# Relaying the orders of three engines and the places of woven attention pairs in a fused attention and two-FFN kernel

## The reference, cut to what matters

```python
def _attn_ref(q, k, v):                       # q, k, v: (8, 8, 576, 64)
    ...                                       # nine chunks of 64 rows for each head
    scores = scale * np.matmul(q_c, k_c.transpose(0, 1, 2, 4, 3))
    scores = scores - np.max(scores, axis=-1, keepdims=True)
    attn = np.exp(scores)
    attn = attn / (np.sum(attn, axis=-1, keepdims=True) + 1e-09)
    out = np.matmul(attn, v_c)

def _moe_ref(x, w_gate, w_val, w_out, rms_g): # x: (4608, 512), F = 1536
    rms = np.sqrt(np.mean(x * x, axis=-1, keepdims=True) + 1e-06)
    xn = x / rms * rms_g
    g = xn @ w_gate
    silu = g * (1.0 / (1.0 + np.exp(-g)))
    return (silu * (xn @ w_val)) @ w_out

def _moe2_ref(x, w_in, w_out):                # F = 2048
    h = x @ w_in
    g = h * np.clip(h + 3.0, 0.0, 6.0) / 6.0
    return g @ w_out
```

## Time and profile before

| | us |
|---|---|
| median of 3 runs | 1653.3 |
| lowest, highest | 1642.41, 1655.88 |
| the profiled execution, its own time | 1644.85 |
| its span | 1643.1 |

### The profile page before, as it was taken

One profiled execution on the slowest core, in us unless ns is written; L12 is line 12 of the kernel. 1 busy time (PEld: TensorE's weight loads), 2 busy tenths in 40 slices (PEclk: granted clock), 3 DMA queues, 4 the chain that ended last, 5 costly groups with the idle time before them and its releaser, 6 DMA issues.

```text
span 1643.1 us, 29732 instructions
## 1 busy us (share of the span) xinstructions
PE 1603.6 (98%) x11335; PEld 1568.2 (95%) x11337; DVE 1046.2 (64%) x1441; ACT 858.8 (52%) x1341; POOL 783.7 (48%) x774
## 2 busy tenths in 40 slices
PE   7899999999999999999999999999999999999998
PEld 5688999899999999999999999999999999999998
DVE  4878877868754446755454776665666865455454
ACT  4666766654644444644444565554655654434432
POOL 2543442459876564423240377777676631231231
PEclk9999999999999999999999999999999999999999
DMA  9777777644565655989987856647658986776674
GB/s 181 156 191 170 173 188 168 162 131 155 175 233 198 207 194 197 373 308 315 309 309 279 299 209 239 230 174 251 220 183 287 378 269 202 218 229 212 212 228 118
DMA packets 335646, 366.88 MB, mean 223 GB/s; under 512 B 186256, under 2 KB 299152, under 8 KB 332304
## 3 DMA queue, kind: packets, MB, share of 16 engines
q1 hardware_dynamic: 321584, 334.69, 64.8%
q0 software_dynamic: 8800, 28.85, 5.1%
q10 hardware_dynamic: 5120, 1.44, 0.5%
HBM read 200.80 MB, written 164.10 MB: 222 GB/s over the span
## 4 chain that ended last, share of the span: by engine, by line
PE 86%; SPq 4%; DMA 2%; DVE 2%; issue 2%; POOL 2%; ACT 2%; DVEq 0%; ACTq 0%; POOLq 0%
PE bx L989 14%; PE by L989 14%; PE by L990 14%; PE by L991 14%; PE bx L990 14%; PE bx L991 14%; DMA hl_b<-h_scratch 2%; SPq L583 1%; SPq L576 1%; PE att L958 1%; PE att L967 1%; PE att L914 1%; DVE tx L1523 1%; PE att L937 1%; SPq L590 0%
## 5 line engine op out<-in xcount | busy, mean ns | idle before, releaser
L989 PE MATMUL by<-tx,wr 128*128 128x384 f32 x840 | 285.4, 340 | 4.1 <-ACT vb L1201 2.5
L989 PE MATMUL bx<-tx,wr 128*128 128x384 f32 x840 | 285.5, 340 | 2.6 <-ACT gb L1201 1.2
L991 PE MATMUL bx<-tx,wr 128*128 128x384 f32 x840 | 281.0, 335 | 0.0
L991 PE MATMUL by<-tx,wr 128*128 128x384 f32 x840 | 280.9, 334 | 0.0
L990 PE MATMUL bx<-tx,wr 128*128 128x384 f32 x840 | 280.8, 334 | 0.0
L990 PE MATMUL by<-tx,wr 128*128 128x384 f32 x840 | 280.8, 334 | 0.0
L1574 DVE TENSOR_TENSOR hl_d<-hl_d 128x1536 fp32r<-128x1536 f32 x84 | 147.4, 1788 | 90.1 <-ACT hl_d L1273 90.1
L1892 POOL DMA_DIRECT2D out_dram<-ot x128 | 70.4, 558 | 248.1 <-DVE ot L1597 245.6
L1574 DVE TENSOR_TENSOR hl_b<-hl_b 128x1152 fp32r<-128x1152 f32 x84 | 117.5, 1414 | 106.7 <-ACT hl_b L1273 106.2
L1273 ACT ACTIVATE hl_d<-hl_d 128x1536 fp32r<-128x1536 f32 x84 | 123.3, 1486 | 112.6 <-DMA hl_d<-u_scratch 112.6
L989 PEld LDWEIGHTS by<-tx,wr 128*128 128x128 f32 x840 | 157.7, 188 | 7.6 <-issue 2.8
(11 more groups left out here) (200 smaller groups left out, 3769.6 us busy)
## 6 DMA issues: line engine op xcount, KB each, us to landing
hl_d<-u_scratch SPq DMA_DIRECT2D x84, 768.0 KB, 4.4
hl_b<-h_scratch SPq DMA_DIRECT2D x84, 576.0 KB, 5.8
u_scratch<-ut SPq DMA_DIRECT2D x48, 576.0 KB, 3.7
h_scratch<-ht SPq DMA_DIRECT2D x36, 576.0 KB, 3.5
u_scratch<-ub SPq DMA_DIRECT2D x96, 192.0 KB, 2.7
u_scratch<-ub SPq DMA_DIRECT2D x48, 384.0 KB, 2.5
h_scratch<-vb SPq DMA_DIRECT2D x72, 192.0 KB, 3.2
h_scratch<-vb SPq DMA_DIRECT2D x36, 384.0 KB, 3.1
```

The costliest lines, as they stand in the source:

```text
L989: pe.matmul(dst, w_hi, m_hi, start=start, stop=False, skip_group_check=not opens)
L991: return pe.matmul(dst, w_lo, m_hi, start=False, stop=stop, skip_group_check=not opens)
```

## The change

What TensorE does before the first product is kept. The orders of ScalarE, VectorE and GpSimd around it are relaid; so are the places of pairs 6 to 17, the tables of weight units 2 to 5 and of the operand fills. Unit 3's remainder goes from VectorE to GpSimd. In all woven pairs the shift of the scores stands one slot later and the norm one slot earlier. Loads of q and k for the later pairs start three slots later. In the first lines of SyncE's program q and k of pairs 8 and 9 go ahead of both V loads, and unit 2's raw weights ahead of one V load and of a store.

```diff
--- before.py
+++ after.py
@@ -324,7 +324,7 @@
         return 4 * m + place + 1 if m < B0 else 4 * B0 + 8 * (m - C0) + 2 * place + st + 1
 
 
-    V_C, V_C_SLOT = 11, 28
+    V_C, V_C_SLOT = 11, 27
 
     def qk_buf(n):
         n2 = n // 2
@@ -340,10 +340,10 @@
         return (qk_a, qk_c, qk_b)[which], n % 2 * D, (q_loaded[which], full), (k_loaded[which], full)
 
 
-    QK_FIRST = {5: (5, 2), 6: (10, 2), 7: (27, 2), 8: (41, 2)}
+    QK_FIRST = {5: (3, 2), 6: (9, 2), 7: (27, 4), 8: (44, 4), 9: (56, 4)}
 
     def qk_slots(n2):
-        first, each = QK_FIRST.get(n2, (at_slot_of(2 * n2 - 4, SC) + 4, 1))
+        first, each = QK_FIRST.get(n2, (at_slot_of(2 * n2 - 4, SC) + 7, 1))
         return [first + i // each if i < 14 else first + i - 14 if each == 1 else first + i // each for i in range(16)]
 
     def v_buf(n):
@@ -367,12 +367,12 @@
 
         return 3 * f - 1 if f <= 12 else C0 + 4 * (f - 12) - 1
 
-    SECOND_FILL = {8: 0, 10: 1, 14: 2, 15: 3, 16: 4, 21: 5, 22: 6}
+    SECOND_FILL = {6: 0, 11: 1, 13: 2, 16: 3, 17: 4, 20: 5, 22: 6}
 
     def filled_at(f, slot):
 
 
-        at_slot = SECOND_FILL if f == 1 else {4: 0, 10: 1, 11: 2, 16: 3, 18: 4, 20: 5, 22: 6} if f < 6 else {3: 0, 5: 1, 7: 2, 9: 3, 11: 4, 13: 5, 15: 6}
+        at_slot = SECOND_FILL if f == 1 else {5: 0, 8: 1, 12: 2, 14: 3, 17: 4, 19: 5, 21: 6} if f < 6 else {3: 0, 5: 1, 7: 2, 9: 3, 11: 4, 13: 5, 15: 6}
         return at_slot.get(slot)
 
 
@@ -458,8 +458,8 @@
 
 
     S_FIRST = NG
-    EARLY = {6: (-6, -3, 1, 7), 7: (0, 3, 8, 12), 8: (7, 9, 14, 20), 9: (12, 15, 21, 24), 10: (18, 23, 26, 31), 11: (24, 28, 33, 37), 12: (32, 37, 39, 44), 13: (40, 43, 46, 50), 14: (45, 49, 52, 57), 15: (51, 56, 59, 63), 16: (58, 62, 64, 68), 17: (63, 68, 70, 76)}
-    AFTER = {7: 5, 8: 1, 11: 5, 12: 5, 25: 5, 20: 1, 24: 1, 33: 1, 29: 5, 30: 1, 15: 5, 17: 3, 18: 3, 23: 5, 32: 5, 28: 3, 13: 3, 26: 3, 16: 3, 22: 1, 34: 1, 19: 5, 21: 5, 27: 3}
+    EARLY = {6: (-6, -3, 5, 7), 7: (2, 5, 9, 12), 8: (7, 11, 14, 21), 9: (14, 18, 22, 25), 10: (20, 25, 28, 32), 11: (26, 32, 33, 36), 12: (34, 37, 40, 45), 13: (40, 42, 47, 51), 14: (46, 48, 53, 57), 15: (49, 53, 59, 63), 16: (55, 62, 64, 69), 17: (64, 67, 71, 75)}
+    AFTER = {7: 5, 8: 5, 11: 5, 12: 3, 25: 3, 20: 3, 24: 5, 33: 5, 29: 5, 30: 5, 15: 3, 17: 3, 18: 3, 23: 5, 32: 3, 28: 5, 13: 3, 26: 3, 16: 5, 22: 5, 34: 3, 19: 5, 21: 3, 27: 3, 6: 1, 9: 3, 14: 3, 10: 1, 31: 3}
     SC, TR, AT, XX = 0, 1, 2, 3
 
     def at_slot_of(n, piece):
@@ -505,21 +505,22 @@
         return sum(16 * 8 * len(runs_out(s, a)) for s in range(NSB) for a in range(2) if s % 2 == parity and s // 2 < times)
 
 
-    FIRST_SUMS = {4: XT3, 9: XT4}
-    FIRST_HI = {3: 4, 8: 6}
-    FIRST_LO = {6: 4, 8: 6}
-    SECOND_SUMS = {9: XT1, 10: XT2, 12: XT3, 13: XT4}
+    FIRST_SUMS = {3: XT3, 7: XT4}
+    FIRST_HI = {7: 4, 9: 6}
+    FIRST_LO = {7: 4, 10: 6}
+    SECOND_SUMS = {7: XT1, 11: XT2, 12: XT3, 13: XT4}
 
 
     RAW_AT = {6: (14, 9), 7: (14, 10), 8: (16, 11), 9: (16, 13), 10: (18, 11), 11: (18, 13), 12: (19, 12), 13: (20, 2), 22: (34, 0)}
-    RAW_FIRST_AT = {3: (0, 0), 4: (0, 8), 5: (1, 1)}
-    SUMS_AT = {2: (0, 1), 3: (0, 9), 4: (0, 12), 5: (1, 5), 6: (15, 9), 7: (15, 11), 8: (17, 1), 9: (17, 9), 10: (19, 1), 11: (19, 4)}
-    HI_AT = {2: ((0, 3), (0, 4)), 3: ((0, 9), (0, 10)), 4: ((1, 2), (1, 2)), 5: ((1, 9), (1, 11)),
+    RAW_FIRST_AT = {3: (0, 0), 4: (0, 7), 5: (0, 13)}
+    SUMS_AT = {2: (0, 2), 3: (0, 9), 4: (1, 0), 5: (1, 7), 6: (15, 9), 7: (15, 11), 8: (17, 1), 9: (17, 9), 10: (19, 1), 11: (19, 4)}
+    HI_AT = {2: ((0, 2), (0, 3)), 3: ((0, 8), (0, 11)), 4: ((1, 0), (1, 2)), 5: ((1, 8), (1, 10)),
              6: ((16, 2), (16, 3)), 7: ((16, 4), (16, 6)), 8: ((18, 7), (18, 8)), 9: ((18, 9), (18, 10)),
              10: ((19, 6), (19, 7)), 11: ((19, 8), (19, 9))}
-    LO_AT = {2: ((0, 6), (0, 6)), 3: ((0, 9), (0, 12)), 4: ((1, 4), (1, 4)), 5: ((1, 11), (1, 13)),
+    LO_AT = {2: ((0, 2), (0, 6)), 4: ((1, 4), (1, 4)), 5: ((1, 11), (1, 12)),
              6: ((16, 3), (16, 5)), 7: ((16, 6), (16, 8)), 8: ((18, 8), (18, 9)), 9: ((18, 10), (18, 12)),
              10: ((19, 7), (19, 8)), 11: ((19, 9), (19, 10))}
+    LO_POOL_AT = {3: ((0, 9), (0, 12))}
     STAGE_AT = {}
     U_B = 21
     for u in range(UB, U_B + 1):
@@ -753,11 +754,11 @@
                 load_first_v(n // 2 - 1)
             if n in (5, 7):
                 load_raw_a((n - 5) // 2)
+        load_qk(4)
         load_v(NG)
+        load_raw_a(2)
         load_v(NG + 1)
-        load_qk(4)
         store_x(0, 0)
-        load_raw_a(2)
 
         for m in range(0, 18):
             s, j = m // 3, m % 3
@@ -1333,19 +1334,19 @@
                 weight_hi(0, n - 3)
             if n == 5:
                 fill_hi(0, 0)
+        norm_rows(S_FIRST - 2)
+        weight_hi(1, 0)
+        mean_square(S_FIRST - 1)
         copy_k(S_FIRST + 1)
+        norm_rows(S_FIRST - 1)
         exponentials(S_FIRST)
-        norm_rows(S_FIRST - 2)
-        mean_square(S_FIRST - 1)
-        weight_hi(1, 0)
-        norm_rows(S_FIRST - 1)
+        weight_hi(1, 1)
+        fill_hi(0, 5)
         fill_hi_early(1)
-        fill_hi(0, 5)
+        fill_hi(0, 1)
+        fill_hi(0, 2)
         copy_probsT(S_FIRST)
-        weight_hi(1, 1)
-        fill_hi(0, 1)
         fill_hi_early(2)
-        fill_hi(0, 2)
         fill_hi(0, 3)
 
         for m in range(B0):
@@ -1364,7 +1365,7 @@
                 n = woven(m, slot, AT, 2)
                 if n is not None:
                     mean_square(n)
-                n = woven(m, slot, AT, 4)
+                n = woven(m, slot, AT, 3)
                 if n is not None:
                     norm_rows(n)
                 n = woven(m, slot, SC, 2)
@@ -1532,6 +1533,8 @@
             if u == 1 and part == 0:
 
                 dve.wait_ge(w_lo, part_no(0, 1))
+            if u - 1 in LO_POOL_AT and part == 0:
+                dve.wait_ge(w_lo, part_no(u - 1, 1))
             dve.wait_ge(w_hi, part_no(u, part))
             dve.tensor_tensor(dst[:, :, LO], blocks_of(u, part), dst[:, :, HI].bitcast(F32), ALU.subtract).then_inc(w_lo, 1)
 
@@ -1634,17 +1637,17 @@
             if n > 0:
                 scale_attention(n - 1)
         shift_scores(S_FIRST)
-        copy_q(S_FIRST + 1)
+        fill_lo(0, 0)
         evict_x(S_FIRST - 3)
         scale_attention(S_FIRST - 1)
-        fill_lo(0, 0)
         evict_x(S_FIRST - 2)
+        copy_q(S_FIRST + 1)
         weight_lo(1, 0)
+        evict_x(S_FIRST - 1)
+        weight_lo(1, 1)
+        fill_lo(0, 5)
         fill_lo_early(1)
-        evict_x(S_FIRST - 1)
-        fill_lo(0, 5)
         fill_lo(0, 1)
-        weight_lo(1, 1)
         fill_lo_early(2)
         fill_lo(0, 2)
         fill_lo(0, 3)
@@ -1660,14 +1663,15 @@
                     gated(m - 1, H21)
                 if m > 0 and slot == 1:
                     gated(m - 1, H11)
+                n = woven(m, slot, SC, 1)
+                if n is not None and n + 1 < NN and next_transposed_after(n) == 1:
+                    transpose_qk(n + 1)
+                n = woven(m, slot, SC, 2)
+                if n is not None:
+                    shift_scores(n)
                 n = woven(m, slot, AT, 1)
                 if n is not None:
                     scale_attention(n)
-                n = woven(m, slot, SC, 1)
-                if n is not None and n + 1 < NN and next_transposed_after(n) == 1:
-                    transpose_qk(n + 1)
-                if n is not None:
-                    shift_scores(n)
                 if m > 0 and slot == 3:
                     gated(m - 1, H22)
                 if m > 0 and slot == 4:
@@ -1796,6 +1800,8 @@
 
         def weight_lo(u, part):
             dst = parts_to(u, part)
+            if u > 0 and part == 0:
+                pool.wait_ge(w_lo, part_no(u - 1, 1))
             pool.wait_ge(w_hi, part_no(u, part))
             pool.tensor_tensor(dst[:, :, LO], blocks_of(u, part), dst[:, :, HI].bitcast(F32), ALU.subtract).then_inc(w_lo, 1)
 
@@ -1905,15 +1911,15 @@
         inverse_rms(1)
         sums(0)
         inverse_rms(2)
+        inverse_rms(3)
         weight_lo(0, 0)
         weight_lo(0, 1)
-        inverse_rms(3)
+        inverse_rms(4)
         sums(1)
-        inverse_rms(4)
+        x_sum_early(XT1)
         inverse_rms(5)
-        x_sum_early(XT1)
+        x_sum_early(XT2)
         x_sum(0, XT1)
-        x_sum_early(XT2)
         x_sum(0, XT2)
 
         for m in range(B0):
@@ -1939,6 +1945,8 @@
                     x_sum(f, slot - 8)
                 for u in units_at(SUMS_AT, m, slot):
                     sums(u)
+                for u, part in parts_at(LO_POOL_AT, m, slot):
+                    weight_lo(u, part)
                 if m == B0 - 2 and slot in (1, 4):
                     pool.wait_ge(prod, prod_no(m - 1, 6, 1))
                     load_block(0, slot // 4)
```

## The result

The changed kernel took 1643.5 us in the median of 21 runs (1639.4 to 1650.4), the kernel before 1650.0 in 21 runs beside it (1642.4 to 1655.9). The ratio is 0.9958, with a 95% interval of 0.9947 to 0.9969: a gain of 5 to 9 us. Two profiled executions can't show it: this one of the changed kernel took 1645.49 (span 1643.7), and the one of before 1644.85 (span 1643.1), a quick draw of its kernel. So spans are no guide here; I compare stretches between the same product slots.

What follows compares the result with a forecast made beforehand. TensorE, busy 98% of the span, was taken as the bound, leaving 39.5 us of idle. Step 0 (-2.2), steps 1 to 5 (-0.6) and 6 to 17 (-4.5) sum to -7.3 from a mean of 1649.1: 1642 us, range 1631 to 1655.

Steps and rivals of the forecast that it cites:

- Steps 6 to 17: Later blocks: new fill, norm and shift places remove waits on rows, evictions and accumulators; gain 4.5 us, bounds -5.6 and +2.
- I leave 1.1 for what is late next: Steps 6 to 17: of 5.6 us of idle addressed, 1.1 was kept for the next late thing.
- the transpose at slot 12: Steps 6 to 17: nearest new victim if operand 1's early rounding holds ScalarE up to 1.9 us; over one us spare.
- Step 0: First woven step: stalls removed against new costs, ending 2.2 us early; bounds -5 to +2.
- The two plain stalls: Step 0: TensorE's 2.55 us before slot 7 and 1.00 before pair 8's probabilities, both to go.
- Term (2): Step 0, slot 2: operand 1's remainder behind a split part, start 53.7 instead of 53.13, a loss of 1.9 us.
- Term (3): Step 0, pair 7's probabilities: unit 2's sums from 53.7, remainder 58.8, transpose 60.8; 0.6 us late at slot 6.
- Steps 1 to 5: Pairs' new distances: idle falls from 5.2 to 4.6 us, pair 13 worst at 1.4; gain 0.6, bounds -4 and +4.
- (a): Rival, steps 0 to 17: nearly all addressed idle clears, only four floors remain; -14 us, 1635; chance 0.20.
- (b): Rival: only the later part pays, step 0 gives nothing, steps 1 to 5 lose; -2 us, 1647; chance 0.13.
- (c): Rival: weight chain bounds step 0 if unit 2's sums end after about 59 us; +5 us, 1654; chance 0.10.
- (d): Rival, whole change: moved orders are off the chain except at named stalls; 0 within 1 us, 1649; chance 0.07.

Runs made afterwards that it cites:

- before_again: The kernel before, unchanged, profiled a second time; 1647.3 us in its one run.
- late_only: The kernel before with only the parts of the change that act from step 6 on; 1646.5 us, ratio 0.9985 to the kernel before.
- fill1_10: The changed kernel with operand 1 of blocks 2 to 5 rounded at slot 10 instead of 8; 1639.6 us, ratio 0.9956 to the kernel before.
- unit2_later: The changed kernel with weight unit 2's rounding and remainder moved from slots 2 and 3 to 4 and 5; 1641.2 us, ratio 0.9962 to the kernel before.
- clock run: unit2_later with ten filler matmuls ahead of the attend of slot 1, to keep TensorE busy; 1640.5 us, ratio 0.9966 to the kernel before.
- fill5_later: The changed kernel with operand 5's rounding and remainder behind operand 3's instead of ahead of operand 1's; 1641.4 us, ratio 0.9972 to the kernel before.
- tr13_44: The changed kernel with the transpose of pair 13's probabilities at slot 44 instead of 42; 1641.4 us, ratio 0.9953 to the kernel before.
- best: The changed kernel with fill5_later, fill1_10, tr13_44 and pair 9's rows transposed one slot later; 1640.3 us, ratio 0.9971 to the kernel before.
- after_again: The changed kernel, unchanged, run once more; 1641.4 us, ratio 0.9971 to the kernel before.
- both_later: The changed kernel with the moves of both unit2_later and fill5_later; 1642.3 us, ratio 0.9977 to the kernel before.

## Why the prediction was right, and where it was not

**The number.** 1642 was forecast and 1643.5 measured; the gain over the kernel before beside it was 6.5 us against 7.3. Most of the parts behind it came out smaller: the traces place 3.2 us of it, so that the number came this near is in part luck. Of the signs of being wrong one came, pair 7's transpose later than 62. TensorE's idle in steps 0 to 5 was 10.1 us, under the 12.4, and it waited for no transfer. "The clock is no lever here" was read off one trace; before_again and late_only, with the old order in step 0, have half clock there.

**Steps 6 to 17: -4.5 forecast, -3.2 measured**, in every trace that has them. The mechanism held: the longer waits on rows went and so did the late evictions (one of 0.3 us is left). The step that failed is "I leave 1.1 for what is late next"; it was 2.4. I had looked for it at "the transpose at slot 12"; it came at slot 13 of steps 8 and 11, on a combination behind the remainder. fill1_10 shows it by taking 2.1 us away. The cause I had named, operand 1's early rounding, was right; its victim was VectorE's combination, not ScalarE's exponential.

**Step 0: -2.2 forecast; -0.54 in the first traces of the two kernels and -0.35 in the second.** The forecast holds the 0.5 of a later slot 0, so for the step's own length it is -2.7. The two plain stalls went as said, but the 2.55 us was dear only in some executions: it was 1.29 in before_again and 0.95 in late_only, where the slots ahead of it had run at half clock. Term (2), slot 2 at 53.7, was 54.57. VectorE's timeline of the kernel after, ahead of it:
```profile
51.03 1.50 DVE L1524 TENSOR_TENSOR tx<-xr,tx 128x768 fp32r<-128x768 f32 x1
52.45 1.21 DVE L1529 TENSOR_TENSOR tx<-xt,tx 128x512 fp32r<-128x512 f32 x1
53.57 0.94 DVE L1524 TENSOR_TENSOR tx<-xt,tx 128x256 fp32r<-128x256 f32 x1
...
58.24 2.47 DVE L1539 TENSOR_TENSOR wr<-w_raw_a,wr 128x1024 fp32r<-128x1024 f32 x1 [0.31 <-ACT wr L1187]
```
Term (3) had pair 7's transpose at 60.8. The sums began at 53.07 (53.7 forecast) and the remainder at 58.24, but it took 2.47 us where I had reckoned 1.2, having begun inside a GpSimd sum (57.39 to 59.63); in unit2_later, with GpSimd idle, it took 1.22. The transpose came at 62.75, past the 62 that I had given as wrong. The row of 2.11 us that bears on this stood in the earlier trace rows, and I let it weigh on operand 6 alone. The Trainium skill, SBUF — State Buffer, Who interferes with whom, lets a VectorE operation with both inputs in SBUF and a GpSimd one that reads SBUF exclude each other; the runs agree, with 1.21 against 2.84 us for one remainder. And slots 2 and 3, which I had priced at full clock, took 4.5 us; but the clock run shows that at full clock there the next wait takes most of that back. Slot 8 came at 67.23, not 65.4, and step 1 at 76.39, not 75. So the term of this part that failed is the remainder's length in (3), 1.2 for 2.47.

**Steps 1 to 5: -0.6 forecast, -0.35 here, +0.9 against before_again: nothing shown.** The clock blurs it. Without a stretch at half clock these steps took 104.6 to 104.8 us in three traces with the changed tables (unit2_later, fill5_later, tr13_44) and 105.4 to 106.6 in three with the old ones; with one they took 106.0 to 106.4 in six traces with the changed tables and 106.4 in one with the old. Pair 13 stood 2.02 us against 1.4 forecast; its row is below. Pair 9's rows stood 1.83 against 0.6, where the longest such wait in the earlier trace rows was 0.9; that is the term of this part that was mis-sized most. ScalarE's timeline of the kernel after there:
```profile
91.57 1.06 ACT L1187 ACTIVATE wr<-w_raw_a 128x1024 fp32r<-128x1024 f32 x1 [0.43 <-POOL w_sum_a L1799]
92.54 0.58 ACT L1153 ACTIVATE att<-xn 128x513 f32<-128x513 f32 x1
...
93.15 0.83 ACT L1187 ACTIVATE wr<-w_sum_a 128x768 fp32r<-128x768 f32 x1
94.94 0.72 ACT L1158 ACTIVATE xn<-xn,inv_rms 128x512 f32<-128x512 f32 x1 [0.96 <-POOL inv_rms L1889]
```
The mean square stands behind a weight rounding, and the norm then waits for GpSimd's inverse root. In best, which transposes these rows one slot later, it is gone; 1.36 us before pair 11's scores stand in its place. Against that, steps 4 and 5 gave 1.7 us, more than I had allowed them. At pair 13, ScalarE's timeline of the kernel after, behind the last silu, which ends at 120.64:
```profile
120.54 0.83 ACT L1173 ACTIVATE tx<-xt 128x768 fp32r<-128x768 f32 x1
121.38 0.60 ACT L1153 ACTIVATE att<-xn 128x513 f32<-128x513 f32 x1
121.92 0.19 ACT L1153 ACTIVATION_READ_ACCUMULATOR att<-xn 128x1 f32 x1
122.12 1.28 ACT L1139 ACT_TABLE_LOAD   x1
123.42 0.63 ACT L1139 ACTIVATE pr<-pr 128x512 f32<-128x512 f32 x1
```
My 1.9 us from the silus to the end of the exponential left out a rounding and a mean square that stand between; it was 3.4. The table load itself takes 1.28 us, starts 0.01 us behind the operation ahead of it, and the exponential starts 0.02 us behind its end. The Trainium skill, ScalarE: Activation LUTs, What ACT_TABLE_LOAD costs, has a drain of 1.38 us beside the load; the trace doesn't agree, the time beside it is ScalarE's own work.

**What isn't placed.** The first product came at 46.3 us in the mean of ten traces with the new order ahead of it (45.6 to 47.1) and at 45.6 in the mean of four with the old one (45.4 to 46.2): a loss of 0.7 where I had forecast 0.5. In sum the traces place -3.2 us in steps 6 to 17, and step 0 and the first product cancel each other. The times say -6.5 (-5 to -9), and -4.8 (-2 to -8) beside after_again. The rest, 1.6 to 3.3 us, stays open: it is smaller than what the code behind slot 252 varies by. One part of that variation is seen. VectorE's timeline of the kernel after in a step of the second FFN, then of the kernel before at the same slot:
```profile
983.53 1.81 DVE L1524 TENSOR_TENSOR tx<-xt,tx 128x768 fp32r<-128x768 f32 x1
```
```profile
987.15 0.94 DVE L1523 TENSOR_TENSOR tx<-xt,tx 128x768 fp32r<-128x768 f32 x1
```
A pair of steps with such crossings with GpSimd's work takes 1.1 us longer (30.2 against 29.1). There are four such pairs in this trace of the changed kernel and none in its second, none in the first trace of before and two in its second. So they belong to the execution, not to the order of the code, as far as these traces tell.

**The rivals.** (a), that nearly all clears, is out: TensorE still stands 2.83, 1.83 and 2.02 us. (b), only the later part pays, is nearest to what the traces show, and with -3.2 for its -2 it is the better account of the mechanism, though the measured time is nearer the forecast's. (c), the weight chain, is half true: sums of unit 2 ended at 57.1, before the 59 from which it decides, and the chain was late all the same, in the remainder behind them. (d) is out by late_only.

## What to carry to other kernels

Before an elementwise remainder is moved on VectorE, look at what GpSimd does at its new time: here it cost either its own length or that plus most of what was left of GpSimd's (1.21 or 2.84 us), and a shift of 0.1 us can decide, so that such a place should be given room rather than be aimed at. Tables for all blocks pay the same in each execution and can be read in one trace; a start-up of a few slots can't, and wants stretches between equal slots, in two traces of each kernel. In four of the six attempts at a stall (unit2_later, both_later, clock, tr13_44) another wait took its place, so follow the queue behind it before giving it a price. And look at the clock of the whole step in more than one trace, not only where it first fell.

## What was not expected of the hardware

Where the clock fell to 0.50 in steps 0 to 5, TensorE had stood 1.7 to 3.8 us just before. Around slot 2 it was at 0.50 in each of the six traces where TensorE stood 2.83 us, and at 1.00 where it stood 1.44 or where fillers ran; but in the four traces without it there, it fell behind the next long idle, of 2.19 to 3.78 us. Each of the ten traces with the new order has half clock somewhere in step 0; with the old order two of four have it, behind idles of 2.46 and 2.48 us, and two have full clock behind the same idles. Before pair 13, the same idle of 2.02 us was followed by half clock in some executions and not in others; TensorE's stretches of fill1_10 and of the kernel after, from 124 to 126 us:
```profile
124.00:126.00 2.00, 2.00 (x9) 0.50 0.79 122
```
```profile
124.00:126.00 2.00, 1.90 (x13) 1.00 0.81 126
```
It costs 1.57 us each time (24.63 against 23.06 in step 3). In late_only it fell there behind 1.70 us, and behind the 1.83 us before pair 9's rows only in the first trace of the changed kernel. What else decides it was not found. And the time of a whole stretch of unchanged code, some 1240 us long, spread by 8 us over fourteen traces, in which the starting order of VectorE and GpSimd is one visible part.
